# Seven products for eight in the first output tile of a second layer, with sums on GpSimd

## The chip, the cores and the metric

The kernel runs on one core of one Trainium2 chip. The metric is the device time of the whole program in microseconds. The engines are PE (TensorE), DVE (VectorE), ACT (ScalarE), GpSimd (POOL) and SP (SyncE, which issues nearly all DMAs here).

## The reference

```
kv  = k^T v per head;  a = q kv                  # (4, 8, 576, 64), no softmax
x   = a / rms(a) * g_norm                        # then tokens x features: 2304 x 512
x   = ((x @ w_a) * (x @ w_b)) @ w_out            # layer 1, d_ff = 1536
out = (sigmoid(x @ w_gate) * (x @ w_val)) @ w_out2   # layer 2, same sizes
```

All is fp32. The kernel splits each matmul operand in a high part (fp32r) and a low part (the rest) and adds three passes: high x high, high x low, low x high.

## The kernel before, in words

Each layer runs over three tiles of 768 tokens: tiles 0, 1, 2 are layer 1, tiles 3, 4, 5 are layer 2. The first products (x with w_a and w_b) go by a scheme that makes a 2 x 2 block product with seven multiplications instead of eight, for which sums and differences of blocks of both operands are needed. Such a tile has 12 units (v = 0 to 11), each 256 columns of one of the two weight matrices. A unit is seven products on PE (`product`, line 991, 6 matmuls each: two chunks by three passes), drained by ACT (lines 1262, 1281, 1288, 1295, 1423) and DVE (lines 1548, 1554, 1778, 1814, 1820, 1831). Meanwhile ACT (line 1220) and DVE (line 1608) split the weights of the next unit in high and low parts, four groups each. In tiles 0 and 3 the weights are fresh: DVE also makes their sums (line 1574, four instructions per unit) and SP spills them to DRAM; later tiles load them.

PE takes a unit's products in the order 0 to 6. Product 6 waits for `c22_ready`, which DVE's line 1548 gives after product 4. So line 1548 must end before product 5 is through, or PE waits.

The outputs (h with w_out) are made in two ways. `fast(tau)` is true for tiles 1, 2, 4 and 5. There they go by seven products as well (`output_product`), 42 steps of h, with sums of blocks of h on DVE (lines 1662, 1666, 1669, 1673) and stored sums of w_out. Tiles 0 and 3 make them directly (`project`): 24 steps of 9 matmuls, in tile 3 with 512 columns each. In tile 3 the first of these steps are put behind the units' products. While tile 3 does so, it also loads w_out, splits it (ACT line 1242, DVE line 1621) and spills the parts to `wo_dram`, for the tiles after it.

The sums of w_out are made in six jobs a layer (`sum_wo`, line 1638, four DVE instructions on 256 columns; then a split by ACT, line 1253, and DVE, line 1644; then a spill of 1 MB). The table says at the end of which unit each starts:

```
SUMS_AT = ({6: 0, 8: 1, 10: 2}, {1: 3, 3: 4, 5: 5}, {}, {3: 0, 5: 1, 7: 2, 9: 3}, {1: 4, 4: 5}, {})
```

So layer 1's are in tiles 0 and 1, layer 2's in tiles 3 and 4. Their stage is the buffer `t_raw`, which also holds the sums over the tokens' blocks (`sum_tokens`, line 1602, four DVE instructions on 768 columns). These are made in units 8 to 11 of each tile for the next one.

The order of work on every engine is written out by hand: each engine runs its queue in order and waits on semaphores. GpSimd has small steps of the normalisation in tile 0 (lines 838 to 844) and nothing after it.

Of the kernel before, what the change touches and what calls it, by code (L numbers as in the profile page):

```python
# [12 lines left out]
P = 128  # L13
# [3 lines left out]
def attention_and_two_layers(nc, q_in_dram, k_in, v_in, g_norm, layer_weights, out):  # L17
# [83 lines left out]
    with ExitStack() as ctx:  # L101
# [128 lines left out]
        wo_sums_spilled = sem("wo_sums_spilled")  # L230
        stored = [sem(f"stored{i}") for i in range(3)]
# [64 lines left out]
        def fast(tau):  # L296
            return tau % TILES != 0

        def fast_index(tau):
            return tau - tau // TILES - 1  # L300
# [26 lines left out]
        def steps_behind(tau, v):  # L327

            if fast(tau):
                return ()  # L330
            if tau:
                return (v - 2,) if v >= 2 else ()
            return (2 * (v - OUT_FROM), 2 * (v - OUT_FROM) + 1) if v >= OUT_FROM else ()

        def steps_split(tau, v):

            return (v - 1,) if tau else steps_behind(tau, v + 1)
# [80 lines left out]
        def all_wo_spills(layer, slot):  # L418
            return sum(1 for i, (tau, k) in enumerate(WO_USES)
                       if i % WO_RING == slot and fresh_step(tau, k) and tau <= layer * TILES)  # L420
# [46 lines left out]
        def wait_h_slot(eng, tau, q):  # L467
# [3 lines left out]
            elif tau and fast(tau - 1):  # L471
                wait_projected(eng, tau - 1, FAST_STEPS - H_RING + q)
            elif tau and q < H_RING_DIRECT:
                wait_projected(eng, tau - 1, DIRECT_STEPS - H_RING_DIRECT + q)
            elif tau:

                eng.wait_ge(wo_sums_spilled, 16 * PAIRS * (tau // TILES + 1))
# [75 lines left out]
        SUMS_AT = ({6: 0, 8: 1, 10: 2}, {1: 3, 3: 4, 5: 5}, {}, {3: 0, 5: 1, 7: 2, 9: 3}, {1: 4, 4: 5}, {})  # L553
# [8 lines left out]
        def wo_sum_job(tau, p):  # L562
            return tau // TILES * PAIRS + p
# [21 lines left out]
        def store_run(eng, tc, column, run):  # L585
# [3 lines left out]
                          out_sb[first:first + p1 - p0, tc, column:column + DH_OUT]).then_inc(stored[tc], 16)  # L589

        @block.sync
        def _(sp):
# [65 lines left out]
            def load_wo_sum_raw(tau, p):  # L658
                job = wo_sum_job(tau, p)
                if p:  # L660
                    sp.wait_ge(wo_sum_ready, 4 * job)
                else:
                    sp.wait_ge(x_lo_ready, 7 * tau + 7)
                if fast(tau):
                    sp.wait_ge(wo_lo_ready, CHUNKS * (tau // TILES + 1))
                for odd in range(2):
                    m = 2 * p + odd
                    sp.dma_start(wo_sum_raw(tau, p)[:, 2 * odd:2 * odd + 2, :],
                                 layer_weights[tau // TILES][2][m * P:(m + 1) * P, :].rearrange("p (d n) -> p d n", d=2)
                                 ).then_inc(wo_sum_raw_loaded, 16)  # L670

            def spill_wo_sums(tau, p):
                sp.wait_ge(wo_sum_lo_ready, 2 * wo_sum_job(tau, p) + 2)
                sp.dma_start(wo_sums_dram[tau // TILES, :, :, p, :, :].rearrange("s p n d -> p s (n d)"),
                             wo_sum_parts().rearrange("p s n d -> p s (n d)").bitcast(F32)).then_inc(wo_sums_spilled, 16)

            def load_wo(tau, k):
# [4 lines left out]
                if fast(tau):  # L682
                    if k == 0:
                        for i in range(WO_RING):
                            sp.wait_ge(wo_spilled[i], 16 * all_wo_spills(layer, i))
# [60 lines left out]
            for tau in range(ALL_TILES):  # L746
                if tau:
                    store(tau - 1, 0 if fast(tau - 1) else 1)
                for v in range(UNITS):
                    u = unit(tau, v)  # L750
                    spill_sums(u + 1)
                    if fast(tau):
                        if v - 1 in SUMS_AT[tau] and SUMS_AT[tau][v - 1] < PAIRS - 1:
                            load_wo_sum_raw(tau, SUMS_AT[tau][v - 1] + 1)
                        if v - 2 in SUMS_AT[tau]:
# [3 lines left out]
                        if 6 <= v < 6 + WO_RING:  # L759
# [25 lines left out]
                if fast(tau):  # L785
# [4 lines left out]
                    load_wo_raw(tau + 1, 0)  # L790
# [31 lines left out]
        def _(pool):  # L822
# [9 lines left out]
            for s in range(ALL_STEPS):  # L832
                z, done = s % 2, POOL_STEPS * s
                pool.wait_ge(sum_ready, s + 1)
                if s >= 2:
# [9 lines left out]
                                   ).then_inc(pool_steps, 1)  # L845

        @block.tensor
        def _(pe):
# [189 lines left out]
            def output_product(tau, i):  # L1038
# [6 lines left out]
                for c, a in sorted(order, key=lambda ca: ca[1] // 2) if by_banks else order:  # L1045
# [23 lines left out]
                    at = slice(a * P, (a + 1) * P)  # L1069
                    for n_pass, (hh, part) in enumerate(((h_hi, 0), (h_hi, 1), (h_lo, 0))):  # L1070
# [82 lines left out]
        def _(act):  # L1153
# [91 lines left out]
            def split_wo_sums(tau, p):  # L1245
                job = wo_sum_job(tau, p)
                act.wait_ge(wo_sum_ready, 4 * (job + 1))
                if p:
                    act.wait_ge(wo_sums_spilled, 16 * job)
                elif tau > 1:  # L1250
# [162 lines left out]
            for tau in range(ALL_TILES):  # L1413
                layer = tau // TILES
                for v in range(0 if tau else 1, UNITS):
# [11 lines left out]
                    if not b_unit and v and tau and not fast(tau):  # L1427
                        split_h(tau, v - 1)
# [10 lines left out]
                    if v == UNITS - 1 and not fast(tau):  # L1439
                        split_outs(tau, steps_split(tau, v))  # L1440
# [6 lines left out]
                    if tau == 0 and v < UNITS - 1:  # L1447
                        split_outs(tau, steps_split(tau, v))
# [5 lines left out]
                    elif tau and v < UNITS - 1 and v:  # L1454
                        split_wo(tau, v - 1)
                        if b_unit:
# [449 lines left out]
```

## Time and profile before

| | us |
|---|---|
| median of three runs | 882.55 (880.62 to 883.23) |
| the profiled execution | 879.22 |
| its span in the trace | 877.0 |
| busy in the span: PE, DVE, ACT, GpSimd | 862.5, 648.3, 514.4, 19.4 |
| tile 2, products and outputs | 336.4 to 467.6 |
| tile 3, products and direct outputs | 467.6 to 606.8 |
| tile 4, products and outputs | 606.8 to 740.4 |

Starts are counted from the start of the span. Durations of matmuls overlap, since they are pipelined; the distance between starts is what counts, and the chain of work gives it. DVE's instructions overlap by some 0.08 us as well.

### The profile page before, as it was taken

Reading aid. Unit: us, or ns where it says so; the run is one execution under the profiler, and the core shown is the slowest. Engines: PE = TensorE matmul, PEld = TensorE weight load, DVE = VectorE, ACT = ScalarE, POOL = GpSimd, SP = SyncE. Lnnn points to the kernel's source line nnn. Section 1 sums busy time; section 2 is a strip of 40 time slices with the busy share of each in tenths; the row PEclk is TensorE's granted clock in tenths of the full one; section 3 lists DMA queues with packets and bytes.
Section 4 is the critical chain, followed back from the end, with each engine's and each line's share of the span. In section 5 each row is a group of like instructions: output and inputs, shape, how many; then the busy total and the mean of one; then the engine's idle time right before and its main releaser. Section 6 shows DMA issues by size and latency. Waiting matters only on the chain.

```text
span 877.0 us, 16391 instructions
## 1 busy us (share of the span) xinstructions
PE 862.5 (98%) x5844; PEld 835.5 (95%) x5844; DVE 648.3 (74%) x1272; ACT 514.4 (59%) x1044; POOL 19.4 (2%) x69
## 2 busy tenths in 40 slices
PE   6999999999999999999999999999999999999998
PEld 4889999999999999999999999988999999999998
DVE  4987788864888884768985888983787894676673
ACT  5856665554665674555675556563666584656453
POOL 1111110000000000000000000000000000000000
PEclk9999999999999999999999999999999999999999
DMA  9782258995777681445683588888646586445276
GB/s 346 246 297 77 95 184 314 318 323 183 240 213 268 200 296 58 144 168 193 201 276 122 181 293 279 280 288 288 209 163 253 181 293 171 150 139 199 94 240 195
DMA packets 99508, 189.81 MB, mean 216 GB/s; under 512 B 6884, under 2 KB 49124, under 8 KB 99428
## 3 DMA queue, kind: packets, MB, share of 16 engines
q1 hardware_dynamic: 99348, 188.71, 63.7%
q8 instruction: 47, 0.77, 0.4%
q14 instruction: 33, 0.27, 0.1%
q10 hardware_dynamic: 80, 0.07, 0.0%
HBM read 146.28 MB, written 42.47 MB: 215 GB/s over the span
## 4 chain that ended last, share of the span: by engine, by line
PE 94%; DMA 2%; DVE 2%; ACT 1%; SPq 1%; issue 1%; POOLq 0%; POOL 0%; DVEq 0%; ACTq 0%
PE psum L991 59%; PE psum L1077 10%; PE psum L1075 10%; PE psum L1030 5%; PE psum L1027 5%; PE psum L911 2%; DMA q_in<-in_q_dram 1%; PE psum L929 1%; PE psum L868 1%; DMA wo<-wo_dram 1%; PE psum L888 1%; SPq L597 0%; ACT kv L1163 0%; DVE t_raw L1638 0%; DVE h_parts L1654 0%
## 5 line engine op out<-in xcount | busy, mean ns | idle before, releaser
L991 PE MATMUL psum<-x_hi,w_hi 128*128 128x384 f32 x1008 | 341.6, 339 | 0.6 <-DVE h L1548 0.4
L991 PE MATMUL psum<-x_hi,w_lo 128*128 128x384 f32 x1008 | 338.4, 336 | 0.0
L991 PE MATMUL psum<-x_lo,w_hi 128*128 128x384 f32 x1008 | 337.9, 335 | 0.0
L991 PEld LDWEIGHTS psum<-x_hi,w_hi 128*128 128x128 f32 x1008 | 189.4, 188 | 5.9 <-issue 2.4
L991 PEld LDWEIGHTS psum<-x_lo,w_hi 128*128 128x128 f32 x1008 | 189.5, 188 | 2.3
L991 PEld LDWEIGHTS psum<-x_hi,w_lo 128*128 128x128 f32 x1008 | 189.3, 188 | 0.0
L1313 ACT ACTIVATE h_parts<-h 128x384 fp32r<-128x384 f32 x178 | 92.6, 523 | 78.0 <-PE psum L1077 25.6
L1608 DVE TENSOR_TENSOR w_lo<-s_raw,w_hi 128x512 fp32r<-128x512 f32 x144 | 98.6, 686 | 49.5 <-ACT w_hi L1220 49.2
L1608 DVE TENSOR_TENSOR w_lo<-w_raw,w_hi 128x512 fp32r<-128x512 f32 (+1 forms) x144 | 79.4, 552 | 71.3 <-ACT w_hi L1220 71.3
L1654 DVE TENSOR_TENSOR h_parts<-h,h_parts 128x384 fp32r<-128x384 f32 x178 | 96.7, 553 | 22.6 <-ACT h_parts L1313 22.3
L1077 PE MATMUL psum<-wo,h_parts 128*128 128x256 f32 x756 | 91.0, 283 | 0.0
L1077 PEld LDWEIGHTS psum<-wo,h_parts 128*128 128x128 f32 x756 | 91.0, 192 | 0.0
L1262 ACT ACTIVATE psum<-psum 128x384 f32<-128x384 f32 x72 | 34.2, 475 | 95.4 <-PE psum L991 94.5
L1220 ACT ACTIVATE w_hi<-s_raw 128x512 fp32r<-128x512 f32 x144 | 86.8, 626 | 1.8 <-DVE s_raw L1574 1.8
L1075 PE MATMUL psum<-h_parts,wo 128*128 128x384 f32 x504 | 87.7, 334 | 0.0
L1075 PEld LDWEIGHTS psum<-h_parts,wo 128*128 128x128 f32 x504 | 87.4, 188 | 0.0
L1220 ACT ACTIVATE w_hi<-w_raw 128x512 fp32r<-128x512 f32 (+1 forms) x144 | 74.5, 517 | 1.3 <-DMA w_raw<-in_moe_w_a_dram 1.3
L1030 PE MATMUL psum<-wo,h_parts 128*128 128x512 f32 x216 | 58.2, 393 | 0.8 <-DVE wo L1621 0.5
L1027 PE MATMUL psum<-h_parts,wo 128*128 128x384 f32 x288 | 54.5, 336 | 0.4 <-DVE wo L1621 0.2
L1027 PEld LDWEIGHTS psum<-h_parts,wo 128*128 128x128 f32 x288 | 50.1, 188 | 1.4 <-DMA wo<-wo_dram 0.9
L1423 ACT ACTIVATE c_a<-psum 128x384 f32<-128x384 f32 x36 | 17.7, 492 | 53.9 <-PE psum L991 53.9
L1030 PEld LDWEIGHTS psum<-wo,h_parts 128*128 128x128 f32 x216 | 39.7, 188 | 6.6 <-DVE wo L1621 1.5
(101 smaller groups left out, 816.3 us busy)
## 6 DMA issues: line engine op xcount, KB each, us to landing
wo<-wo_dram SPq DMA_DIRECT2D x60, 512.0 KB, 5.2
s_raw<-s_dram SPq DMA_DIRECT2D x48, 512.0 KB, 4.6
wo<-wo_sums_dram SPq DMA_DIRECT2D x48, 512.0 KB, 4.4
s_dram<-s_raw SPq DMA_DIRECT2D x24, 512.0 KB, 4.5
wo_dram<-wo SPq DMA_DIRECT2D x24, 512.0 KB, 5.2
wo_sums_dram<-h_parts SPq DMA_DIRECT2D x12, 1024.0 KB, 7.4
w_raw<-in_moe_w_a_dram SPq DMA_DIRECT2D x18, 512.0 KB, 3.5
w_raw<-in_moe_w_b_dram SPq DMA_DIRECT2D x18, 512.0 KB, 3.5
```

Of the source, the lines that this page charges most:

```text
L911: last = pe.matmul(to, qT[:, s % 2, at:at + ROWS], heads, start=True, stop=True, tile_position=(0, half * ROWS))
L991: last = pe.matmul(to[:, 0:HT], w[:, u % 2, at, c, :], xx[:, i, c, :], start=(OPENS[i] and c == 0 and n_pass == 0), stop=(c == 1 and n_pas ...
L1027: last = pe.matmul(acc_bank[a][:, 0:HT], wo[:, slot, a // 2, part, at], hh[:, h_slot(tau, q), :], **flags)
L1030: last = pe.matmul(acc_bank[a][:, :].rearrange("p (d n) -> p d n", d=2), hh[:, h_slot(tau, q), a * P:(a + 1) * P], wo[:, slot, :, part, :] ...
L1075: last = pe.matmul(to, wo[:, slot, q % 2, part, at], hh[:, h_slot(tau, q), :], **flags)
L1077: last = pe.matmul(to, hh[:, h_slot(tau, q), at], wo[:, slot, q % 2, part, :], **flags)
L1220: act.activation(split_of(w_hi, u, g), w_groups(u)[g], ACT.Copy).then_inc(w_hi_ready, 1)
L1262: act.activation(product_bank(u, BANK_B)[:, 0:HT], product_bank(u, BANK_A)[:, 0:HT], ACT.Copy).then_inc(seed_ready, 1)
L1313: act.activation(h_hi[:, h_slot(tau, q), :], h_raw(tau, q), ACT.Copy).then_inc(h_hi_ready, 1)
L1423: act.activation(c_a[:, 1, :], product_bank(u - 1, BANK_B)[:, 0:HT], gate(tau)).then_inc(c21_a_ready, 1)
L1608: dve.tensor_tensor(split_of(w_lo, u, g), w_groups(u)[g], split_of(w_hi, u, g).bitcast(F32), ALU.subtract).then_inc(w_lo_ready, 1)
L1654: dve.tensor_tensor(h_lo[:, h_slot(tau, q), :], h_raw(tau, q), h_hi[:, h_slot(tau, q), :].bitcast(F32), ALU.subtract).then_inc(h_lo_ready, 1)
```

## The change

`fast(tau)` becomes `tau > 0`, so tile 3 makes its outputs by seven products too. The parts and sums of layer 2's w_out must then exist before tile 3's outputs, and are made in tiles 2 and 3. Each of the six jobs now has two more steps, which make the parts of the two chunks of w_out themselves: ACT copies 1024 columns (`split_wo_blocks`) and GpSimd subtracts (1024 columns); the parts stand in the first two slots of the ring `wo` and are spilled from there. `sum_wo` for layer 2 moves from DVE to GpSimd, and `sum_tokens` for tiles 3 and 4 too. The split of the sums stays on ACT and DVE. The loads of parts for the outputs of tiles 2 and 3 start at units 9 to 11 instead of 6 to 10. One matmul of 512 columns is added, which opens a PSUM bank at the start of tile 3's outputs.

```diff
         def fast(tau):
-            return tau % TILES != 0
+            return tau > 0
...
-        SUMS_AT = ({6: 0, 8: 1, 10: 2}, {1: 3, 3: 4, 5: 5}, {}, {3: 0, 5: 1, 7: 2, 9: 3}, {1: 4, 4: 5}, {})
+        SUMS_AT = ({6: 0, 8: 1, 10: 2}, {1: 3, 3: 4, 5: 5}, {0: 0, 2: 1, 4: 2, 6: 3}, {1: 4, 5: 5}, {}, {})
...
+        def sum_wo(eng, tau, p):
...
+                if i == 0:
+                    eng.wait_ge(wo_sum_raw_loaded, 32 * (job + 1))
+                    if job:
+                        eng.wait_ge(wo_sum_lo_ready, 2 * job)
+                    eng.wait_ge(x_lo_ready, 7 * tau + 7)
+                elif i >= 2:
+                    eng.wait_ge(wo_sum_ready, 4 * job + (1, 3)[i - 2])
+                eng.tensor_tensor(to, in0, in1, op).then_inc(wo_sum_ready, 1)
...
+                if tau:
+                    eng.wait_ge(x_lo_ready, 7 * tau)
+
+                    if fast(tau - 1):
+                        eng.wait_ge(wo_sum_lo_ready, 2 * sums_until(tau - 1))
...
             def load_wo_sum_raw(tau, p):
                 job = wo_sum_job(tau, p)
-                if p:
+                if job:
                     sp.wait_ge(wo_sum_ready, 4 * job)
...
+                if sums_layer(tau) and p:
+                    sp.wait_ge(wo_block_lo_ready, p)
...
+            def spill_wo_blocks(p):
+                sp.wait_ge(wo_block_lo_ready, p + 1)
+                for odd in range(2):
+                    sp.dma_start(wo_dram[1, :, odd, :, p, :].rearrange("d p n -> p d n"),
+                                 wo_block_parts()[:, odd].rearrange("p d s n -> p d (s n)").bitcast(F32)).then_inc(wo_blocks_spilled, 16)
...
+                        if tau == 1 and v == 7:
+                            load_wo_sum_raw(2, 0)
+                        if sums_layer(tau) and SUMS_AT[tau]:
+                            for k in {9: (0,), 10: (1, 2), 11: (3, 4)}.get(v, ()):
+                                load_wo(tau, k)
+                        elif 6 <= v < 6 + WO_RING:
...
+            for tau in range(2, 4):
+                for p in SUMS_AT[tau].values():
+                    sum_wo(pool, tau, p)
+                    pool.wait_ge(wo_block_hi_ready, p + 1)
+                    pool.tensor_tensor(wo_block_parts()[:, :, :, 1, :], wo_raw[:, :, :].rearrange("p o (d n) -> p o d n", d=2),
+                                       wo_block_parts()[:, :, :, 0, :].bitcast(F32), ALU.subtract).then_inc(wo_block_lo_ready, 1)
+                for i in range(4):
+                    sum_tokens(pool, tau + 1, i)
...
+                    if tau == TILES and i == 0 and c == 0 and a == 0:
+
+                        pe.matmul(bank[OUT_BANKS[BANK_B][0]][:, :].rearrange("p (d n) -> p d n", d=2),
+                                  h_hi[:, h_slot(tau, 0), at], wo[:, slot, :, 0, :], start=True, stop=True)
...
+            def split_wo_blocks(tau, p):
+                act.wait_ge(wo_sum_raw_loaded, 32 * (wo_sum_job(tau, p) + 1))
+                if p:
+                    act.wait_ge(wo_blocks_spilled, 32 * p)
+                if first_sum(tau, p):
+
+                    act.wait_ge(acc_done, acc_before(tau, 0))
+                act.activation(wo_block_parts()[:, :, :, 0, :], wo_raw[:, :, :].rearrange("p o (d n) -> p o d n", d=2),
+                               ACT.Copy).then_inc(wo_block_hi_ready, 1)
...
-                    if 0 < tau < ALL_TILES - 1 and v >= 8:
-                        sum_tokens(tau + 1, v - 8)
+                    if tau in (1, 4) and v >= 8:
+                        sum_tokens(dve, tau + 1, v - 8)
```

## Rows read from the trace of the kernel before

**Rows 1.** Stretches: length; busy PE, PEld, DVE, ACT, GpSimd; clock; DMA share, GB/s.
```profile
336.40:467.60 131.20, 131.20 (x758) 130.97 (x757) 98.42 (x185) 76.00 (x156) 0.00 (x0) 1.00 0.53 179
467.60:606.80 139.20, 138.41 (x722) 128.48 (x721) 106.22 (x209) 80.11 (x155) 0.00 (x0) 1.00 0.74 255
606.80:740.40 133.60, 133.41 (x884) 132.60 (x883) 100.93 (x190) 81.39 (x163) 0.00 (x0) 1.00 0.64 215
740.40:873.60 133.20, 133.13 (x882) 132.41 (x881) 85.16 (x162) 73.61 (x152) 0.00 (x0) 1.00 0.54 170
```

**Rows 2.** The chain that ended last: start, length, what.
```profile
336.41 87.54 PE psum L991 x504
423.95 43.68 PE psum L1075 x252
...
580.00 26.84 PE psum L1030 x117
...
695.04 45.36 PE psum L1077 x378
740.39 87.79 PE psum L991 x504
```

**Rows 3.** DVE in order of time, tile 2, around the start of unit 2.
```profile
351.70 0.42 DVE L1608 TENSOR_TENSOR w_lo<-w_raw,w_hi 128x256 fp32r<-128x256 f32 x1
352.04 0.55 DVE L1778 TENSOR_TENSOR h<-psum,c_a 128x384 f32<-128x384 f32 x1
353.14 0.69 DVE L1608 TENSOR_TENSOR w_lo<-w_raw,w_hi 128x512 fp32r<-128x512 f32 x1 [0.55 <-ACT w_hi L1220]
353.75 0.55 DVE L1654 TENSOR_TENSOR h_parts<-h,h_parts 128x384 fp32r<-128x384 f32 x1
355.22 0.69 DVE L1608 TENSOR_TENSOR w_lo<-s_raw,w_hi 128x512 fp32r<-128x512 f32 x1 [0.92 <-ACT w_hi L1220]
355.83 0.55 DVE L1662 TENSOR_TENSOR h<-h 128x384 f32<-128x384 f32 x1
356.30 0.55 DVE L1548 TENSOR_TENSOR c_a<-psum,c_a 128x384 f32<-128x384 f32 x1
```

**Rows 4.** ACT's last copy of tile 2's unit 2; DVE's weight sums in tile 3.
```profile
356.12 0.41 ACT L1220 ACTIVATE w_hi<-w_raw 128x256 fp32r<-128x256 f32 x1
...
475.56 0.76 DVE L1574 TENSOR_TENSOR s_raw<-w_raw 128x256 f32<-128x256 f32 x2
...
477.06 0.69 DVE L1608 TENSOR_TENSOR w_lo<-w_raw,w_hi 128x512 fp32r<-128x512 f32 x1
```

**Rows 5.** The only wait of PE's matmuls in tile 4; the chain beneath it.
```profile
PE psum L991 <- DVE c_a L1548: 0.2, 1, 0.2
638.82 1.10 DVE t_raw L1638 x3
```

**Rows 6.** DVE and GpSimd (POOL) side by side in tile 0.
```profile
68.67 0.68 DVE L1608 TENSOR_TENSOR w_lo<-s_raw,w_hi 128x512 fp32r<-128x512 f32 x1
68.84 0.56 POOL L838 TENSOR_SCALAR half_mean<-sum_sq 128x8 f32<-128x8 f32 x1 [10.03 <-DVE sum_sq L1502]
...
73.26 0.75 DVE L1574 TENSOR_TENSOR s_raw<-w_raw 128x256 f32<-128x256 f32 x2
73.43 0.30 POOL L841 TENSOR_TENSOR inv_sq<-inv 128x8 f32<-128x8 f32 x1 [0.62 <-DVE inv L1510]
...
83.98 0.55 DVE L1778 TENSOR_TENSOR h<-psum,c_a 128x384 f32<-128x384 f32 x1
84.16 0.20 POOL L838 TENSOR_SCALAR half_mean<-sum_sq 128x8 f32<-128x8 f32 x1 [5.11 <-DVE sum_sq L1502]
```

**Rows 7.** Groups by line, GpSimd's fills and ACT's split of sums (busy, mean ns).
```profile
L824 POOL MEMSET kv<- 128x1024 f32 x2 | 1.8, 952 | 0.3 <-POOLq L1890 0.3
L1253 ACT ACTIVATE h_parts<-x 128x1024 fp32r<-128x1024 f32 x7 | 7.3, 1048 | 0.0
```

**Rows 8.** DMA issues: tile, queue, count, size, median us to landing.
```profile
w_raw<-in_moe_w_gate_dram SPq DMA_DIRECT2D x18, 512.0 KB, 3.5
```

More of the change, by code:

```diff
@@ L416, in wo_spills, with all_wo_spills @@
             return sum(1 for i in range(w + 1) if i % WO_RING == w % WO_RING and fresh_step(*WO_USES[i]))
-        def all_wo_spills(layer, slot):
-            return sum(1 for i, (tau, k) in enumerate(WO_USES)
-                       if i % WO_RING == slot and fresh_step(tau, k) and tau <= layer * TILES)
+        def all_wo_spills(slot):
+            return sum(1 for i, (tau, k) in enumerate(WO_USES) if i % WO_RING == slot and fresh_step(tau, k))
         W_GROUP = (slice(4, 6), slice(0, 2), slice(2, 4), slice(6, 7))
@@ L549, in wo_sum_stage, with sums_layer, first_sum, sums_until @@
             return x[:, 0:4, start:start + DH_OUT]
-        SUMS_AT = ({6: 0, 8: 1, 10: 2}, {1: 3, 3: 4, 5: 5}, {}, {3: 0, 5: 1, 7: 2, 9: 3}, {1: 4, 4: 5}, {})
+        SUMS_AT = ({6: 0, 8: 1, 10: 2}, {1: 3, 3: 4, 5: 5}, {0: 0, 2: 1, 4: 2, 6: 3}, {1: 4, 5: 5}, {}, {})
+        def sums_layer(tau):
+            return 0 if tau < 2 else 1
+        def first_sum(tau, p):
+            return p == min(SUMS_AT[tau].values())
+        def sums_until(tau):
+            return sum(len(jobs) for jobs in SUMS_AT[:tau + 1])
         def wo_sum_raw(tau, p):
@@ L589, in store_run, with sum_tokens @@
                           out_sb[first:first + p1 - p0, tc, column:column + DH_OUT]).then_inc(stored[tc], 16)
+        def sum_wo(eng, tau, p):
+            job = wo_sum_job(tau, p)
+            a11_, a21_, a12_, a22_ = [wo_sum_raw(tau, p)[:, n, :] for n in range(4)]
+            s1_, s2_, s3_, s4_ = [wo_sum_stage(tau)[:, n, :] for n in range(4)]
+            for i, (to, in0, in1, op) in enumerate(((s1_, a21_, a22_, ALU.add), (s3_, a11_, a21_, ALU.subtract),
+                                                    (s2_, s1_, a11_, ALU.subtract), (s4_, a12_, s2_, ALU.subtract))):
+                if i == 0:
[6 more added lines that the diff above has]
+                eng.tensor_tensor(to, in0, in1, op).then_inc(wo_sum_ready, 1)
+        def sum_tokens(eng, tau, i):
+            b11, b12 = b_block(tau, 0, 0), b_block(tau, 0, 1)
+            b21, b22 = b_block(tau, 1, 0), b_block(tau, 1, 1)
+            t = [t_raw[:, 0, :, :], t_raw[:, 1, :, :], b12, t_raw[:, 2, :, :]]
+            if i == 0:
+                if tau == 0:
+                    eng.wait_ge(x_ready, FIRST_TILE_STEPS - 1)
+                elif tau < TILES:
+                    eng.wait_ge(x_ready, ALL_STEPS)
+                else:
+                    eng.wait_ge(act_drained, act_before(tau - TILES + 1, 0))
+                    eng.wait_ge(dve_drained, dve_before(tau - TILES + 1, 0))
+                if tau:
+                    eng.wait_ge(x_lo_ready, 7 * tau)
+                    if fast(tau - 1):
+                        eng.wait_ge(wo_sum_lo_ready, 2 * sums_until(tau - 1))
+            if i:
+                eng.wait_ge(t_raw_ready, 4 * tau + (1, 1, 2)[i - 1])
+            if tau == 0 and i == 1:
+                eng.wait_ge(x_ready, FIRST_TILE_STEPS)
+            if tau == 1 and i != 2:
+                eng.wait_ge(h_lo_ready, {0: 6, 1: 8, 3: 10}[i])
+            in0, in1 = ((b12, b11), (b22, t[0]), (b22, b12), (b21, t[1]))[i]
+            eng.tensor_tensor(t[i], in0, in1, ALU.subtract).then_inc(t_raw_ready, 1)
         @block.sync
@@ L1247, in split_wo_sums @@
                 act.wait_ge(wo_sum_ready, 4 * (job + 1))
-                if p:
+                if job:
                     act.wait_ge(wo_sums_spilled, 16 * job)
-                elif tau > 1:
+                if tau > 1 and first_sum(tau, p):
                     for q in range(FAST_STEPS - H_RING + H_RING_DIRECT, FAST_STEPS):
@@ L1792, in _ @@
                     behind(v, 2)
-                    if v in SUMS_AT[tau]:
-                        sum_wo(tau, SUMS_AT[tau][v])
+                    if sums_layer(tau) == 0 and v in SUMS_AT[tau]:
+                        sum_wo(dve, tau, SUMS_AT[tau][v])
                     if fast(tau):
```

152 lines of the change are left out of this document (46 added, 106 removed).

## The prediction

> **What bounds the kernel now.** I read the windows by tile first. In tiles 2, 4 and 5 PE is busy for the whole stretch, in tile 3 for 138.41 of 139.20 us, always at a granted clock of 1.00, which is the 2.4 GHz level [rows 1]. The chain of work that ended last says the same: from tile 1 on it is PE nearly without a break [rows 2]. So the time is the number of PE's matmuls, plus whatever makes PE wait, and other engines count only where they are late for it. DVE is the nearest to being late: 98.42, 106.22 and 100.93 us in tiles 2 to 4 [rows 1]. GpSimd stands at 0.00 in all of them. That idle engine is what the change uses.
>
> **What PE saves.** From the chain: the tile's products are 504 matmuls in 87.54 us (12 units of 7.30, each seven products of 1.04), the outputs by seven products of the second layer are 378 matmuls in 45.36 (0.120 each), a direct one is 26.84 / 117 = 0.229 [rows 2]. Tile 3 runs from 423.95 + 43.68 = 467.63 to 580.00 + 26.84 = 606.84: 139.2 us. After the change it is 87.6 + 45.4 + 0.23 (the matmul that opens the bank) = 133.2. Saved: 6.0. Of them 216 x 0.229 - 45.4 - 0.2 = 3.9 are matmuls, the rest are the small waits of the direct tile, which wait for parts of w_out and their loads; these go away with it. In tile 4 the sums of w_out leave DVE too; there they made PE wait [rows 5], and tile 4's products take 695.04 - 606.84 = 88.2, tile 5's 87.8 [rows 2]: 0.4. Total gain 6.4.
>
> **What is moved at no cost.** ACT gets six copies of 1024 columns for twelve of 512; it is busy for 80 of tile 3's 139 us [rows 1] and is through its work of an even unit 1.8 us before the unit ends [rows 4]. DMA moves the same 6 MB of parts to DRAM, in tiles 2 and 3 instead of 3 alone; 21 loads of parts (512 KB) take the place of 12, over tile 3's outputs, as in tiles 4 and 5, where PE does not wait. SP now waits for GpSimd's low parts before `load_unit(u + 3)` in every second unit of tile 2. Behind it are weights that are used two units later, 14.6 us, and a load lands in 3.5 us [rows 8]; without that cover PE would wait for the whole delay, some 2 us a time. I put all of this at 0.
>
> **What GpSimd costs DVE.** This decides it. The new GpSimd instructions are 24 sums of 256 columns, 6 subtractions of 1024 and 8 sums over 768, all with two SBUF inputs. The trace before has only tiny ones, but they show how the two engines meet. A GpSimd operation on 8 columns takes 0.20, also beside a DVE subtraction with an input in PSUM. Beside a DVE subtraction with both inputs in SBUF it takes 0.56, and ends 0.05 after it. It also got in between two such DVE instructions that stand back to back (73.26 for both, GpSimd's done at 73.73) [rows 6]. So both need something that only one holds, for a whole instruction of DVE, and they take turns. That DVE waits in the same way for a whole instruction of GpSimd is no row: I assume it, since what is shown is one resource taken in turns. The Trainium skill, "SBUF — State Buffer", section "SBUF: two separate sides", states just that: an exclusive lock against DVE instructions with two SBUF inputs, held for a whole instruction by whichever came first, the other fully blocked. The trace agrees for GpSimd's side. By what the row alone proves the change would give its 6.4 us; by the rule it costs what follows.
>
> The price of a GpSimd instruction: a fill of 1024 columns, one stream, takes 0.92 [rows 7], so 0.9 ns a column; the fixed part is 0.20 [rows 6]. A two-input operation moves three streams: between one stream's rate (all overlap) and three's. I take two, 1.8 ns: 0.66 for 256, 1.58 for 768, 2.04 for 1024. The ends are 0.43 / 0.89 / 1.12 and 0.89 / 2.27 / 2.96. The Trainium skill, "GPSIMD Engine Reference", section "Elementwise — side-by-side cycle accounting", has 4497 ns for 2048 fp32 columns, 2.2 ns a column; by it the waits below would sum to 26 and the time to about 902; no run here shows it yet.
>
> Now where they fall. Tile 2, unit 2 starts at 336.41 + 14.6 = 351.0. PE's seventh product needs DVE's line 1548 and starts 6.24 into the unit, 357.24; line 1548 ends at 356.85 [rows 3]: slack 0.4. Before it DVE does four instructions with two SBUF inputs: lines 1608, 1654, 1608, 1662.
> - *Sums, jobs 1 to 3.* `sum_wo` of job p waits until DVE has split the sums of the job before, since they share t_raw. DVE does that at the end of the odd unit: 351.70 + 0.34 + 2 x 0.61 = 353.3. So GpSimd's four instructions of 0.66 start at 353.3 and take turns with just those four of DVE. Taking turns: GpSimd 353.35 to 354.0, line 1608 to 354.7, GpSimd to 355.4, 1654 to 355.95, GpSimd to 356.65, 1608 to 357.35, GpSimd to 358.0, 1662 to 358.6, 1548 to 359.1. PE waits 359.1 - 357.24 = 1.8. In general 4 x (price + 0.05) - 1.0, where the 1.0 is the slack of line 1548 and DVE's own idle time before it. Units 2, 4 and 6: 5.5.
> - *Tokens of tile 3*, four of 1.58, wait for the split of job 3, the same place of unit 8. The same walk gives 4 x 1.63 - 0.9 = 5.6.
> - *Low parts in tile 2*: ACT's last copy of an even unit ends 5.53 into it [rows 3, 4], plus 1.05 for 1024 columns as in line 1253 [rows 7]; GpSimd's 2.04 then lie from -0.7 to +1.4 around the start of an odd unit, in which DVE's next split comes only at 2.1, for ACT is not ready before (as line 1608 at 353.14, 2.14 into unit 2): 0.
> - *Tile 3*: its units are fresh and now 7.30 long, and DVE has four weight sums more in each, 477.06 - 475.56 = 1.50 [rows 4]. By the distances in rows 3 (0.47 for 384 columns, 0.61 for 512, 0.34 for 256) two units are 11 x 0.47 + 6 x 0.61 + 2 x 0.34 + 0.3 for waits on itself = 9.8 us of DVE, with the sums 12.8 of 14.6: it fits, but the idle time in which tile 2 hid the low parts is gone. The two low parts cost 2.04 - 0.4 = 1.6 each: 3.3. The sums of job 5 fall into unit 3, where one of the four runs under work from PSUM: 4 x 0.71 - 1.7 = 1.1. The tokens of tile 4 start about 1 us into unit 7, behind job 5's split, and before line 1548 stand seven instructions with two SBUF inputs; slack 0.8: 4 x 1.63 - 0.8 = 5.7.
> - Sum: 5.5 + 5.6 + 3.3 + 1.1 + 5.7 = 21.2. With the low prices 2.8 + 2.9 + 1.4 + 0.2 + 3.0 = 10.3, with the high ones 8.3 + 8.4 + 5.1 + 2.1 + 8.5 = 32.4. Job 0 and job 4's sums start in the last third of the outputs of the tile before, where DVE has one subtraction (0.47) per step of 1.04: 0.
>
> Net: 21.2 - 6.4 = 14.8 us slower. The profiled execution goes from 879.2 (span 877.0) to 894.0. The three runs shown have their median 3.3 above the profiled one, so I forecast 882.5 + 14.8 = 897.3, and 886.4 (10.3 - 6.4 = 3.9 more) to 908.5 (26.0 more) for this case alone.
>
> **The rivals.**
> - *GpSimd does not hold DVE.* For: no row shows DVE waiting a whole GpSimd instruction, and the two back-to-back sums at 73.26 lost nothing to GpSimd (0.75 there, 0.76 at 475.56 without it) [rows 4, 6]. But those GpSimd instructions read 8 columns, so there was little to lose. Then the 6.4 stay: 876.1. The forecast turns to this side when all waits add up to less than 6.4, so when the jobs hold DVE for less than about a third of what I give them. Chance 0.18.
> - *GpSimd holds DVE only while it reads*, less than the fill's rate makes it. The low sum, less what falls into idle time, is about the gain: 880 to 885. Chance 0.09.
> - *DVE alone is late in tile 3.* 12.8 of 14.6 us leaves 0.9 a unit and DVE must wait for products 4 and 5 at fixed places; missing by 0.5 in each pair of units takes back 3: 879.5. Against: in my schedule line 1548 is ready in time in every fresh unit. As the only effect 0.05; on top of the forecast it is inside the range.
> - *GpSimd is late, not just in the way.* From one job to the next, 14.6 us, GpSimd has 2.96 + 4 x 0.94 = 6.7 us by the high prices, with a load of raw weights between and its own waits for DVE. If that passes 14.6, SP's queue stands behind `wo_block_lo_ready`, weights come late and the loads of w_out at units 9 to 11 as well: 10 or more beyond the forecast. Chance 0.05.
> - *Forecast*: 0.63.
>
> **How the numbers follow.** Within 0.3% is 2.6 us, about what a measurement tells from no change. Faster holds the first rival and the third, 0.23; same, most of the second, 0.08; slower, the rest, 0.69. Both signs carry weight, so the range goes from the first rival, 876, to near the high prices, 905; about 0.15 is left outside.
>
> **What the profile after would show.** GpSimd with 38 instructions in tiles 1 to 3, means near 0.7, 1.6 and 2.0 us or longer when they wait for DVE. DVE's subtractions with two SBUF inputs longer than 0.55 or 0.69, or with gaps before them, just while GpSimd works; lines with a PSUM input unchanged. PE waits for line 1548's semaphore at units 2, 4, 6 and 8 of tile 2 and 2, 6, 7 of tile 3, the longest in tile 2's unit 8 and tile 3's unit 7. Tile 3's outputs 45.4, its products 87.6 plus waits; tiles 4 and 5 without any. The prediction is wrong if DVE's durations do not change beside GpSimd, or if tile 2 stays at 131.2.

## The result and the profile after

The changed kernel takes 899.62 us in the median (896.76 to 901.18, four runs), the kernel before 881.88 beside it (four runs). The ratio is 1.0203, 95% interval 1.0182 to 1.0225: 17.7 us slower. Forecast were 897.3 in a range from 876 to 905, and 14.8 us slower.

The windows by tile (length; busy PE, PEld, DVE, ACT, GpSimd; clock; DMA share, GB/s), which answer to [rows 1]:

```profile
339.50:482.80 143.30, 134.27 (x758) 132.54 (x757) 118.89 (x189) 83.01 (x164) 35.62 (x24) 0.98 0.69 235
482.80:628.80 146.00, 137.68 (x885) 135.16 (x884) 119.41 (x217) 84.28 (x167) 19.20 (x10) 0.98 0.60 204
628.80:762.00 133.20, 133.20 (x884) 132.63 (x883) 95.78 (x177) 79.53 (x162) 0.00 (x0) 1.00 0.58 189
762.00:895.20 133.20, 133.18 (x883) 132.46 (x881) 85.17 (x162) 73.61 (x151) 0.00 (x0) 1.00 0.54 170
```

Tile 2, whose PE work did not change, is 12.1 us longer. DVE is busy 20 us longer there, with four instructions more, so what has grown is mostly the length of its instructions. Tile 3 is not 6 us shorter, but 6.8 longer. Tiles 4 and 5 take 133.2 each, so they have no waits. The chain (start, length, what), against [rows 2], shows where PE stood:

```profile
339.53 17.73 PE psum L1061 x102
...
361.15 4.41 PE psum L1061 x24
...
377.25 4.61 PE psum L1061 x24
...
393.54 4.61 PE psum L1061 x24
...
414.21 24.95 PE psum L1061 x132
439.17 43.68 PE psum L1149 x252
482.85 9.39 PE psum L1061 x54
...
513.92 10.69 PE psum L1061 x60
...
549.41 32.99 PE psum L1061 x174
...
604.81 24.02 PE psum L1151 x198
628.83 87.86 PE psum L1061 x504
```

The pieces of tile 2 begin at the seventh product of units 2, 4, 6 and 8, which waits for the line that was 1548 and is 1628 now. Free of waits the first would begin at 339.53 + 14.6 + 6.26 = 360.4 and the others 14.6 later each. From one piece to the next it is 16.1, 16.3 and 20.67. So PE waits 0.8, then 16.1 - 14.6 = 1.5, 1.7 and 20.67 - 14.6 = 6.1. That is 10.1; the last 2.0 come after it, since 132 matmuls take 24.95 and not the 22.9 of 0.1737 each. What stood in the way in unit 8 is in the order of time, first DVE, then GpSimd:

```profile
404.56 0.55 DVE L1814 TENSOR_TENSOR h<-psum,c_a 128x384 f32<-128x384 f32 x1
405.02 2.18 DVE L1660 TENSOR_TENSOR w_lo<-w_raw,w_hi 128x512 fp32r<-128x512 f32 x1
407.13 2.19 DVE L1690 TENSOR_TENSOR h_parts<-h,h_parts 128x384 fp32r<-128x384 f32 x1
409.24 2.28 DVE L1660 TENSOR_TENSOR w_lo<-s_raw,w_hi 128x512 fp32r<-128x512 f32 x1
411.45 2.15 DVE L1698 TENSOR_TENSOR h<-h 128x384 f32<-128x384 f32 x1
413.52 0.54 DVE L1628 TENSOR_TENSOR c_a<-psum,c_a 128x384 f32<-128x384 f32 x1
...
404.81 1.85 POOL L647 TENSOR_TENSOR t_raw<-x 128x768 f32<-128x768 f32 x1 [9.64 <-DVE h_parts L1680]
406.74 2.17 POOL L647 TENSOR_TENSOR t_raw<-x,t_raw 128x768 f32<-128x768 f32 x1
408.87 2.11 POOL L647 TENSOR_TENSOR x<-x 128x768 f32<-128x768 f32 x1
410.94 2.24 POOL L647 TENSOR_TENSOR t_raw<-x,t_raw 128x768 f32<-128x768 f32 x1
```

Read the two lists as a zip, one instruction from each in turn. GpSimd's first ends at 406.66; DVE's first, issued at 405.02 and normally 0.69 long, ends at 407.20. GpSimd's next ends at 408.91, DVE's, normally 0.55, at 409.32, and so on. A waiting instruction shows as a longer one, not as idle time before it. The first DVE line, with one input in PSUM, runs beside GpSimd's first and keeps its 0.55. (The last, 0.54, begins when GpSimd is through and shows nothing of this.) These are the four turns in just the order that the prediction wrote down.

In tile 3 PE resumes at 513.92, the seventh product of unit 3, 2.9 later than without waits (482.85 + 21.9 + 6.26 = 511.0), and at 549.41, unit 7's, 9.2 later in all. The groups by line (busy, mean ns of one) give GpSimd's prices:

```profile
L912 POOL TENSOR_TENSOR wo<-wo_raw,wo 128x1024 fp32r<-128x1024 f32 x6 | 15.3, 2555 | 56.0 <-ACT wo L1336 56.0
L647 POOL TENSOR_TENSOR t_raw<-x,t_raw 128x768 f32<-128x768 f32 x4 | 8.6, 2144 | 0.2
L619 POOL TENSOR_TENSOR t_raw<-t_raw,wo_raw 128x256 f32<-128x256 f32 x6 | 6.4, 1072 | 0.0
```

These means include GpSimd's own waits for DVE. The shortest single instructions are 2.40 for 1024 columns, 1.85 for 768 and 0.94 for 256, where 2.04, 1.58 and 0.66 were assumed.

And the 2.0 us behind the wait are the clock (same columns as the first windows):

```profile
414.00:416.00 2.00, 1.79 (x6) 1.82 (x7) 1.93 (x5) 0.00 (x0) 0.00 (x0) 0.50 0.00 0
416.00:418.00 2.00, 2.00 (x8) 2.00 (x7) 0.00 (x0) 0.49 (x1) 0.00 (x0) 0.50 0.63 165
418.00:420.00 2.00, 2.00 (x13) 2.00 (x12) 0.58 (x1) 1.50 (x3) 0.00 (x0) 0.96 0.91 357
```

After PE had waited 6.1 us, the granted clock was at half, 1.2 GHz, for some 4.2 us. The same follows unit 7's wait in tile 3: the clock is at 0.50 from 549.4 to 554.7, some 5.3 us, and matmuls start 0.32 apart instead of 0.17. Behind the waits of 1.7 us and less it stayed at 1.00.

### The profile page after: what moved, and what is told of

Its sections match the earlier page's. It is cut to its first block, busy times and chain, and to the rows that moved or that the text cites. A ratio compares the mean times of both kernels' runs of the same rounds, so it can differ in the third digit from the quotient of the medians.

```text
span 899.0 us, 16801 instructions
## 1 busy us (share of the span) xinstructions
PE 867.8 (97%) x6007; PEld 845.7 (94%) x6007; DVE 677.6 (75%) x1272; ACT 523.8 (58%) x1062; POOL 79.4 (9%) x107
## 4 chain that ended last, share of the span: by engine, by line
PE 84%; DVE 8%; DMA 3%; issue 3%; ACT 1%; SPq 1%; POOL 0%; DVEq 0%; ACTq 0%; POOLq 0%
PE psum L1061 50%; PE psum L1151 14%; PE psum L1149 10%; PE psum L1097 5%; DVE w_lo L1660 2%; PE psum L981 2%; DMA wo<-wo_dram 2%; DMA q_in<-in_q_dram 1%; PE psum L938 1%; PE psum L999 1%; DVE s_raw L1654 1%; DVE h L1698 1%; DVE h_parts L1680 1%; DVE h_parts L1690 1%; PE psum L958 1%
## 5 line engine op out<-in xcount | busy, mean ns | idle before, releaser
L1061 PE MATMUL psum<-x_hi,w_hi 128*128 128x384 f32 x1008 | 344.4, 342 | 17.3 <-DVE c_a L1628 10.1
L1660 DVE TENSOR_TENSOR w_lo<-s_raw,w_hi 128x512 fp32r<-128x512 f32 x144 | 109.7, 763 | 55.9 <-ACT w_hi L1294 55.7
L1397 ACT ACTIVATE h_parts<-h 128x384 fp32r<-128x384 f32 x188 | 97.8, 523 | 83.3 <-PE psum L1151 37.6
L1660 DVE TENSOR_TENSOR w_lo<-w_raw,w_hi 128x512 fp32r<-128x512 f32 (+1 forms) x144 | 86.0, 597 | 73.0 <-ACT w_hi L1294 73.0
L1151 PE MATMUL psum<-wo,h_parts 128*128 128x256 f32 x1134 | 136.9, 284 | 0.5 <-DMA wo<-wo_dram 0.5
L1151 PEld LDWEIGHTS psum<-wo,h_parts 128*128 128x128 f32 x1134 | 136.6, 192 | 0.8 <-DMA wo<-wo_dram 0.7
L1690 DVE TENSOR_TENSOR h_parts<-h,h_parts 128x384 fp32r<-128x384 f32 x188 | 105.0, 570 | 19.2 <-ACT h_parts L1397 19.2
L1507 ACT ACTIVATE c_a<-psum 128x384 f32<-128x384 f32 x36 | 17.7, 491 | 60.7 <-PE psum L1061 60.7
L619 POOL TENSOR_TENSOR t_raw<-wo_raw 128x256 f32<-128x256 f32 x12 | 14.8, 1253 | 289.6 <-DVE x_lo L1665 252.8
L1372 ACT ACTIVATE c_a<-psum 128x384 f32<-128x384 f32 x36 | 17.7, 492 | 21.8 <-PE psum L1061 21.7
```

The costliest lines, as they stand in the source:

```text
L1061: last = pe.matmul(to[:, 0:HT], w[:, u % 2, at, c, :], xx[:, i, c, :], start=(OPENS[i] and c == 0 and n_pass == 0), stop=(c == 1 and n_pas ...
L1151: last = pe.matmul(to, hh[:, h_slot(tau, q), at], wo[:, slot, q % 2, part, :], **flags)
L1372: act.activation(h12_home(tau, j) if v % 2 else c_a[:, 2, :], product_bank(u, BANK_B)[:, 0:HT], ACT.Copy).then_inc(u2_ready, 1)
L1397: act.activation(h_hi[:, h_slot(tau, q), :], h_raw(tau, q), ACT.Copy).then_inc(h_hi_ready, 1)
L1507: act.activation(c_a[:, 1, :], product_bank(u - 1, BANK_B)[:, 0:HT], gate(tau)).then_inc(c21_a_ready, 1)
L1660: dve.tensor_tensor(split_of(w_lo, u, g), w_groups(u)[g], split_of(w_hi, u, g).bitcast(F32), ALU.subtract).then_inc(w_lo_ready, 1)
```

## The experiments

All ratios are to the kernel before, measured beside it. "GpSimd does" names its work in tiles 1 to 3. This table has the two tiles that matter, each worked out from the chain's starts as above (tile 2 from its first product to tile 3's, tile 3 to tile 4's):

| kernel | GpSimd does | tile 2 | tile 3 | ratio (95%) |
|---|---|---|---|---|
| before | nothing | 131.2 | 139.2 | 1 |
| the change | sums, low parts, tokens | 143.3 | 146.0 | 1.0203 (1.0182 to 1.0225) |
| small (most of the sums left out) | the same, 8 columns each | 131.3 | 133.7 | 0.9934 (0.9916 to 0.9953) |
| tokens_dve | sums, low parts | 136.8 | 140.6 | 1.0057 (1.0033 to 1.0080) |
| all_dve | nothing | 134.65 | 137.0 | 1.0004 (0.9989 to 1.0018) |
| low_pool | low parts | 136.1 | 139.4 | 1.0039 (1.0024 to 1.0054) |
| moved | nothing | 133.4 | 137.0 | 0.9999 (0.9985 to 1.0013) |
| spread | nothing | 133.75 | 137.9 | 0.9998 (0.9988 to 1.0009) |
| late_sums | nothing | 131.5 | 140.0 | 1.0002 (0.9990 to 1.0013) |
| late_all | nothing | 131.25 | 139.3 | 0.9995 (0.9982 to 1.0008) |
| mixed | nothing | 131.3 | 136.3 | 0.9960 (0.9947 to 0.9973) |

### small: the change without the length of its GpSimd work

```diff
-                    sum_wo(pool, tau, p)
+                    sum_wo(pool, tau, p, 8)
...
-                    sum_tokens(pool, tau + 1, i)
+                    sum_tokens(pool, tau + 1, i, 8)
```

The low part is cut to 8 columns in the same way.

> The changed kernel with each of GpSimd's 38 new instructions cut to 8 columns, all waits, copies, spills and loads in place (so the sums, low parts and token sums of layer 2 are left unmade, and the output is not the reference's). Theory A, GpSimd's long instructions hold DVE: nothing long is left to hold it, tile 2 goes back to 131.2 us, tile 3 to 133.2 to 134.5, and the time is some 6 us below the kernel before, ratio about 0.993. Rival B, DVE is overloaded in tile 3 on its own, whoever makes the sums: tile 2 is free, but tile 3 keeps most of its 12.8 us of extra time, ratio about 1.005. Rival C, DMA traffic or the new waits of SP's queue: both tiles keep their extra time, ratio about 1.02.

Measured: 874.12 us, ratio 0.9934. Its chain from tile 2 to tile 3's outputs has no waits of note:

```profile
336.06 87.62 PE psum L1064 x504
423.68 43.68 PE psum L1152 x252
467.36 20.88 PE psum L1064 x120
488.24 67.26 PE psum L1064 x384
```

The kernel leaves out nearly all of the sums, low parts and token sums of layer 2, so it is a test of time only. The forecast saving is there, tile 3 in 133.7 us where 133.2 were worked out, and nothing of the change but the columns on GpSimd takes it away: not the bank's opening matmul, ACT's copies, the spills, the later loads or SP's waits. Rivals B and C are out. So is the prediction's rival "DVE alone is late in tile 3". This run cannot say whether long GpSimd work hurts by holding DVE or by being late.

### probe: GpSimd work that nobody waits for

Into the kernel before, tile 5:

```diff
+            for at, v in enumerate((2, 4, 6, 8)):
+                pool.wait_ge(product_done, 7 * unit(last, v) + 2)
+                for n in range(4):
...
+                    if v == 2:
+                        op = pool.tensor_tensor(cols[:, 1536:2304], cols[:, 0:768], cols[:, 768:1536], ALU.subtract)
+                    elif v == 4:
+                        op = pool.memset(cols[:, 0:2048], 0.0)
+                    elif v == 6:
+                        op = pool.tensor_copy(cols[:, 1152:2304], cols[:, 0:1152])
+                    else:
+                        op = pool.tensor_tensor(cols[:, 1536:1792], cols[:, 0:256], cols[:, 768:1024], ALU.subtract)
```

> The kernel before with GpSimd instructions that nobody waits for, on the free t_raw in tile 5, four in a row from 2.1 us into a unit: subtractions of 768 columns (unit 2), fills of 2048 (unit 4), copies of 1152 (unit 6), subtractions of 256 (unit 8). Theory A: DVE's instructions with two SBUF inputs get as long as GpSimd's beside the subtractions, and PE waits for line 1548 some 5.5 us in unit 2 and 2 in unit 8, followed by a stretch at half clock in unit 2. The copies read SBUF too and should do the same, 3 to 4.5 us. For the fills no row says; the Trainium skill, SBUF - State Buffer, section on the two separate sides, has DVE's two-input instructions in conflict only with a GpSimd operation that reads SBUF, which would make it 0. Rival, late results and order of work were the cost in the changed kernel: nobody waits here, so tile 5 stays at 133.2.

Measured: 890.49 us (one run), tile 5 in 885.23 - 744.25 = 141.0 for 133.2. In the order of time, GpSimd's four groups, then DVE in unit 2 beside the subtractions, in unit 4 beside the fills, and its line 1672 in unit 6 beside the copies:

```profile
761.12 8.70 POOL L856 TENSOR_TENSOR t_raw<-t_raw 128x768 f32<-128x768 f32 x4 [637.79 <-PE psum L1009]
781.09 7.42 POOL L858 MEMSET t_raw<- 128x2048 f32 x4 [11.27 <-PE psum L1009]
795.72 6.06 POOL L860 COPY t_raw<-t_raw 128x1152 f32<-128x1152 f32 x4 [7.21 <-PE psum L1009]
812.19 4.41 POOL L862 TENSOR_TENSOR t_raw<-t_raw 128x256 f32<-128x256 f32 x4 [10.41 <-PE psum L1009]
...
761.62 2.21 DVE L1672 TENSOR_TENSOR h_parts<-h,h_parts 128x384 fp32r<-128x384 f32 x1
763.75 2.32 DVE L1626 TENSOR_TENSOR w_lo<-s_raw,w_hi 128x512 fp32r<-128x512 f32 x1
765.99 2.15 DVE L1680 TENSOR_TENSOR h<-h 128x384 f32<-128x384 f32 x1
768.07 0.55 DVE L1566 TENSOR_TENSOR c_a<-psum,c_a 128x384 f32<-128x384 f32 x1
...
781.67 0.55 DVE L1672 TENSOR_TENSOR h_parts<-h,h_parts 128x384 fp32r<-128x384 f32 x1
783.15 0.69 DVE L1626 TENSOR_TENSOR w_lo<-s_raw,w_hi 128x512 fp32r<-128x512 f32 x1 [0.92 <-ACT w_hi L1238]
783.75 0.55 DVE L1680 TENSOR_TENSOR h<-h 128x384 f32<-128x384 f32 x1
...
796.31 1.50 DVE L1672 TENSOR_TENSOR h_parts<-h,h_parts 128x384 fp32r<-128x384 f32 x1
```

This settles it. Nobody waits for these instructions, and still DVE's go from 0.55 to 2.2 and PE waits. The fills write SBUF beside DVE for 7.42 us and change nothing (0.55, 0.69); the copies, which read it too, stretch line 1672 to 1.50. So a GpSimd instruction that reads SBUF and a DVE instruction with two SBUF inputs exclude each other here, while a DVE instruction with an input in PSUM is free (0.55 at 768.07, beside the last subtraction). The Trainium skill, "SBUF — State Buffer", section "SBUF: two separate sides", states an exclusive lock with just these conditions, held for a whole instruction; this trace agrees on the conditions, and how much of a recorded length DVE is held for is worked out under "The sizes".

The sizes were off. From the chain PE waits 3.65 in unit 2 (5.5 expected) since DVE's first split was under way when GpSimd's work was issued (761.01 for 761.12) and kept its 0.69, so that DVE was held three times before line 1566 and not four; about 1.5 in unit 6 (3 to 4.5 expected) and 0.6 in unit 8 (2 expected). Half clock after unit 2 costs 1.9.

### tokens_dve: the token sums back on DVE

```diff
-                for i in range(4):
-                    sum_tokens(pool, tau + 1, i)
...
-                    if tau in (1, 4) and v >= 8:
+                    if 0 < tau < ALL_TILES - 1 and v >= 8:
```

> The changed kernel with the token sums of tiles 3 and 4 back on DVE in units 8 to 11, the sums of w_out and the low parts left on GpSimd. Theory A: the two longest waits go, 5.7 in tile 2's unit 8 and 3.9 in tile 3's unit 7, and with them the 2.0 and 2.8 us in which the granted clock is at half behind them. DVE takes eight instructions of 0.95, which fit in tile 2 and cost up to 1.5 in tile 3. About 13 us faster than the changed kernel, ratio to before 1.005 to 1.009. Rival, the work of DVE counts and not who does it: the time stays near 1.02.

Measured: 885.52 us, ratio 1.0057. Tile 2 goes from 143.3 to 136.8: the wait in unit 8 and the slow clock behind it, 8.1, less what DVE's own token sums cost. Tile 3 goes from 146.0 to 140.6. The clock is at 1.00 in both. Eight instructions were some 70% of the loss (0.0146 of 0.0203 in the ratio).

### all_dve and low_pool: who does the rest

all_dve drops GpSimd's loop. It has the token sums on DVE as in tokens_dve, and:

```diff
-                    if sums_layer(tau) == 0 and v in SUMS_AT[tau]:
+                    if v in SUMS_AT[tau]:
                         sum_wo(dve, tau, SUMS_AT[tau][v])
...
+                    if sums_layer(tau) and v in SUMS_AT[tau]:
+                        lower_blocks(tau, SUMS_AT[tau][v])
```

> The changed kernel with everything that it gave to GpSimd on DVE, at the same units: four sums (1.5 us) in the middle of units 0, 2, 4, 6 of tile 2 and 1, 5 of tile 3, the low part (1.15) at the unit's end, token sums in units 8 to 11. Theory A: DVE does each piece in less than half of GpSimd's time and stands still for none of it. Tile 2: the sums come in even units behind the split of the job before, 0.8 us of wait each, about 2.5. Tile 3: 12.8 of 14.6 us of work per two units, plus 7.6 for two jobs and 3.5 for tokens, over by 2 to 5. Ratio 0.997 to 1.002. Rival B, DVE overloaded: more DVE work makes it slower than the changed kernel, ratio over 1.02.

> Everything on DVE as in the run before, but the six low parts (1024 columns) back on GpSimd. Theory A, GpSimd costs what it takes from DVE at that moment: in tile 2 the 2.4 us of a low part fall into the first 2 us of an odd unit, where DVE has nothing ready until ACT's copy, so tile 2 stays at the 134.65 us of the all-DVE kernel or 0.5 below. In tile 3, where DVE has no such idle time, each of the two costs 1 to 1.5 more than DVE's own 1.15: 139 to 140 for 137.0. Ratio to before 1.001 to 1.005. Rival, every GpSimd instruction beside DVE costs PE its length: tile 2 gets 4 x 2.4 longer, ratio over 1.01.

low_pool is all_dve with the six low parts on GpSimd.

all_dve: 880.73 us, ratio 1.0004. DVE has more work, and the kernel is 2% faster than the change by the ratios. Both tiles are near what was expected: tile 2 loses 3.4 (about 2.5 expected), tile 3 3.8 (2 to 5). So the saving of 6 is used up by DVE's own lateness. low_pool: 884.32 us, ratio 1.0039, in the expected range, and so is tile 3 (139.4), but tile 2 missed: 136.1, not 134.65. In the changed kernel the low parts had cost nothing in tile 2, where PE waits only at the sums and token sums. Here they begin at 358.43, behind a line 1548 that is already late, and the split of weights behind it takes 2.68 for 0.68:

```profile
358.43 2.38 POOL L910 TENSOR_TENSOR wo<-wo_raw,wo 128x1024 fp32r<-128x1024 f32 x1 [12.18 <-ACT wo L1332]
...
358.21 0.55 DVE L1624 TENSOR_TENSOR c_a<-psum,c_a 128x384 f32<-128x384 f32 x1
358.67 2.68 DVE L1656 TENSOR_TENSOR w_lo<-s_raw,w_hi 128x512 fp32r<-128x512 f32 x1
```

So a place is free for GpSimd only as long as DVE is not late there for another reason.

### moved and spread: other units

Both have everything on DVE. moved puts tile 2's jobs at odd units and its token sums in units 9 to 11; spread also cuts tile 3's jobs into four pieces, one a unit:

```diff
-        SUMS_AT = (..., {0: 0, 2: 1, 4: 2, 6: 3}, {1: 4, 5: 5}, {}, {})
+        SUMS_AT = (..., {1: 0, 3: 1, 5: 2, 7: 3}, {1: 4, 5: 5}, {}, {})    # moved
+        SUMS_AT = (..., {1: 0, 3: 1, 5: 2, 7: 3}, {0: 4, 4: 5}, {}, {})    # spread
```

> Everything on DVE, tile 2's jobs one unit later, in the odd units 1, 3, 5, 7, token sums in 9 to 11. In an odd unit DVE is idle between its first two splits of weights, so the 1.5 us of sums lie there, and the split of the job before moves to the end of an even unit. Theory: the 3.4 us that tile 2 loses in the all-DVE kernel go down to under 0.5, tile 3 stays at 137.0. Time 2.9 us below the all-DVE kernel, ratio to before 0.995 to 0.998. Rival, the amount of DVE work counts and not its place: no change against 1.000.

> The kernel with moved jobs, and in tile 3 each job spread over four units: two sums, two sums, the low part, the split of the sums, 0.8 to 1.2 us a unit in units 0 to 7, a token sum in each of 8 to 11. DVE has about 0.9 us a unit to spare there (12.8 of 14.6 in two units). Theory: tile 3's 3.8 us of waits shrink to 1 to 2.5, tile 2 as in the moved kernel; ratio to before 0.993 to 0.996. Rival, tile 3 is bound by DVE's total (12.8 x 6 + 11.2 = 88 of 87.6 us): the place does not matter and it equals the moved kernel within 0.5 us.

Both missed: 880.44 us (0.9999) and 881.04 (0.9998). moved's tile 2 is down 1.25 against all_dve, not 2.9 or more. A new wait had come in, in the chain:

```profile
404.75 8.44 DMA wo_sums_dram<-h_parts
```

The last job is one unit later, and so is the spill of its sums. ACT's split of h for ring slot 4 waits 4.7 us for that spill, since the sums' parts lie in slots 4 to 6. ACT's next seed for PE (the copy that PE's second bank starts from) is queued behind it, and PE waits 1.3. spread meets the same (1.5), and its tile 3 is not better (137.9).

### late_sums, late_all, mixed: behind the line that PE waits for

The unit is kept, the place in it is not: the sums go behind line 1548 and the third split. mixed, the last of the three, against all_dve:

```diff
-                    if v in SUMS_AT[tau]:
+                    if tau != 2 and v in SUMS_AT[tau]:
                         sum_wo(dve, tau, SUMS_AT[tau][v])
...
-                    if 0 < tau < ALL_TILES - 1 and v >= 8:
+                    if tau in (1, 4) and v >= 8:
...
+                    if tau == 2 and v in SUMS_AT[tau]:
+                        sum_wo(dve, tau, SUMS_AT[tau][v])
+                    if tau in (2, 3) and v >= 8:
+                        sum_tokens(dve, tau + 1, v - 8)
                     sum_c12(tau, v)
```

late_all has the sums of tile 3 behind the line too: its first condition is `sums_layer(tau) == 0 and v in SUMS_AT[tau]`, its third `sums_layer(tau) and v in SUMS_AT[tau]`. late_sums is that with the token sums ahead of line 1548, those made in tile 2 in units 9 to 11.

> Everything on DVE at the change's units, but the four sums of a job stand behind line 1548 and the third split of weights, just before the second sum of the unit (line 1554's), and tile 3's token sums come in units 9 to 11. What PE waits for next there is the seed of the next unit, some 1.5 us of slack away. Theory, the place against line 1548 decides: tile 2 goes from 134.65 to 131.3 to 132, tile 3 from 137.0 to 136 to 137, since 0.8 per odd unit with a token sum remain; ratio to before 0.995 to 0.998. Rival, the total of DVE's work decides: both as in the all-DVE kernel, 1.000.

> The same, and the token sums for tiles 3 and 4 too stand behind line 1548. Theory: tile 2 131.3 to 132, tile 3 134.5 to 136, ratio to before 0.993 to 0.996. Rival, in tile 3 DVE's total of about 88 us of work in 87.6 us decides: tile 3 stays at 137.

> Everything on DVE; tile 2 as in late_all (sums and token sums behind line 1548), tile 3 with the sums of its two jobs where all_dve has them, before line 1548, and its token sums behind line 1548. Theory, in a tile with fresh weights DVE has no idle time behind line 1548 to catch up in, so the sums cost more there, the short token sums do not: tile 2 131.25, tile 3 136 to 136.6, tiles 2 and 3 together 2.7 to 3.3 less than in the kernel before; ratio 0.995 to 0.998. Rival, tile 3 is bound by the total of DVE's work: 137 or more, ratio 0.998 to 1.000.

Tile 2 came out as expected, 131.5 and 131.25: all of layer 2's preparation there costs at most 0.3 us. Tile 3 did not, 140.0 and 139.3 where 134.5 to 137 were expected, and the gain of tile 2 was lost (880.97 and 880.28 us). mixed was made from that: 876.44 us, ratio 0.9960 (0.9947 to 0.9973), against 880.76 before beside it. Of the kernels that do all the work it is the only one that is clearly faster than the kernel before, by 0.4%. Its chain:

```profile
336.33 87.59 PE psum L1053 x504
423.92 43.68 PE psum L1141 x252
...
603.91 87.87 PE psum L1053 x504
```

Tile 2 is 131.3 and tile 3 is 603.91 - 467.60 = 136.3, as expected.

## Why the prediction was right

**The saving.** 6.0 from the seven products and 0.4 in tile 4 were forecast. Without the length of GpSimd's work tile 3 has 133.7 us for 139.2, 5.5 less, and in the changed kernel tile 4 has 133.2 for 133.6. Right.

**That GpSimd holds DVE for its instruction's length, and that the two take turns.** This was an assumption from instances of the other side [rows 6]. The probe shows it apart from any wait for a result. The rivals "GpSimd does not hold DVE" and "only while it reads, at a fill's rate" are out: 1.5 us for 768 columns, below, is not the 0.89 of a fill's rate. "GpSimd is late" is out too: in tiles 2 and 3 of the changed kernel no wait of DVE, ACT or PE is for a result of GpSimd, and SP waits for one once, 1.3 us, for a spill. In part the success is that of a wide range: from 876 to 905 it held both signs, and the sizes came out close only since errors cancelled.

**The sizes.** By place, forecast and measured: sums in tile 2 5.5 and 4.0 (0.8, 1.5, 1.7); tokens in tile 2 5.6 and 6.1; in tile 3, low parts and sums 4.4 and 5.1, tokens 5.7 and about 4.1. The last comes from the view of PE's waits, which has 3.9 of idle time; 0.17 more hides under the record of the matmul before. The 5.1 are what is left of the 9.2. Sum 21.2 and 19.3. Behind the two low parts only 0.5 and 0.6 are waits for the line, as forecast; 1.2 and 1.0 are waits for ACT's seed, which DVE's lateness holds up:

```profile
PE psum L1061 <- ACT psum L1346: 2.2, 2, 1.2
```

Errors cancelled in this sum. GpSimd's instructions are recorded as 17 to 42% longer than assumed. But their recorded length is not what DVE is held for. In tile 2's unit 2, beside sums of 256 columns:

```profile
358.33 1.20 DVE L1660 TENSOR_TENSOR w_lo<-s_raw,w_hi 128x512 fp32r<-128x512 f32 x1 [0.33 <-ACT w_hi L1294]
359.44 1.09 DVE L1698 TENSOR_TENSOR h<-h 128x384 f32<-128x384 f32 x1
```

They end at 359.53 and 360.53. Of the 1.00 between, 0.55 is line 1698's own, so DVE was held for about 0.45, where the sum's record is 0.94. In the same way the probe's subtractions of 768 columns, whose shortest record in the changed kernel is 1.85, hold DVE for 2.07 - 0.55 = 1.52 (the ends at 766.07 and 768.14). Both are estimates from ends of records. The prediction's walk charged 0.71 and 1.63 a turn. Also, in unit 2 only these two of DVE's four instructions met GpSimd, since the raw weights landed 1.8 us after DVE was ready; in units 4 and 6 all four did.

**The step that was missing** is the clock. I took every wait at its own length. The two long ones were followed by 4.2 and 5.3 us at 1.2 GHz: 2.0 us more in tile 2, and up to 2.8 in tile 3, where 174 matmuls take 32.99 for 30.2. So 19.3 + 4.8 - 6.4 = 17.7 for 21.2 - 6.4 = 14.8. That this is just the medians' difference is luck: the profile's own tiles 2 to 4 give 12.1 + 6.8 - 0.4 = 18.5. The other 0.8 is in tile 3's outputs, 46.2 for 45.4, with a wait for a load of w_out's parts. The probe's tile 4, which its edit does not touch, has 46.1 with the same wait, so this 0.8 is not shown to be the change's.

By the Trainium skill's "GPSIMD Engine Reference", section "Elementwise — side-by-side cycle accounting", at 2.2 ns a column, the time would have been about 902, an estimate. The unhindered 1.85 for 768 and 2.40 for 1024 columns agree with that rate, about 2.15 ns a column over 0.2; the 0.94 for 256 is longer than that gives (0.75).

**Tile 3's own DVE load** was said to fit, and did as long as nothing was added (133.7 for 133.2). What adds to it does cost: all_dve's 11 us of additions 3.3 (137.0 for 133.7), the changed kernel's work on GpSimd 12.3 (146.0 for 133.7), the slow clock included.

**Outside the two tiles.** The changed kernel's profiled span is 22.0 longer, and 3.1 of that lie ahead of tile 1, where the work is the same. The start of tile 1 lies between 204.2 and 209.4 in the profiles of this study, in no order of the kernels, so I take this for the run's and not the change's. It is also why ratios and not single times are used above.

**What stays open.** Why the same sums cost 3.0 more in tile 3 behind line 1548 than ahead of it (late_all 139.3, mixed 136.3, which differ in nothing else). That DVE with fresh weights has no idle time behind the line, and so hands the delay on to the next unit, is argued from its order of work and was not tried by itself.

## What to carry to other kernels

An idle GpSimd is no free help for a VectorE that works on pairs of SBUF tensors. Each of its instructions that reads SBUF can hold up such a VectorE instruction for longer than VectorE would need for the piece itself: about 0.45 us for 0.34 at 256 columns, 1.5 for 0.87 at 768. Look instead for the line that TensorE waits for next, and try the added work just behind it on the same engine. Here that made 14 us of added work in tile 2 nearly free (VectorE busy 112.5 us in the mixed kernel, 98.4 before). It is no rule: in tile 3, whose weights are fresh, the sums cost 3.0 us more behind that line than ahead of it. A wait costs more than its length where it is long enough to bring the clock down.

## What the runs showed that was not expected

- A wait of 3.65 us in the probe's unit 2 was followed by half clock (0.68 and then 0.50 up to 773), waits of 1.7 were not. In these runs the level came back 4 to 5 us later, with PE busy all that time.
- GpSimd's fills of 2048 columns (1.9 us each) and DVE's instructions with two SBUF inputs leave each other's lengths as they are. GpSimd's copies of 1152 columns (6.06 for four, their own waits included) stretch DVE's to 1.5.
- The turns are not strict. In tile 3's unit 7 the first token sum was issued at 540.58 and took 3.01 for 1.85; DVE ran several short instructions back to back before it got its turn.
